# A linear attention's division moved off its matmul result: query features as the moving operand, reciprocals spread over the partitions by DMA

## The chip, the core and the metric

The kernel runs on one core of a Trainium2 chip. The metric is the device time of one execution in microseconds, the median of several runs. The core has five engines with instruction queues of their own: PE (TensorE, matmuls), DVE (VectorE), ACT (ScalarE), POOL (GpSimd) and SP (SyncE, which here only issues DMAs). Each executes its queue strictly in order; between engines the program waits on semaphores.

## The reference

Three stages follow each other. All data are float32; heads have S = 576 tokens of 64 numbers, there are 4 batches of 8 heads.

```
proj = x @ w_phi                         # x = q or k of a head: 576 x 64 -> 576 x 128
proj = proj - max(abs(proj), axis=-1)
phi  = concat(exp(proj), exp(-proj))     # 576 x 256 features
kv   = phi(k).T @ v                      # 256 x 64
z    = sum over tokens of phi(k)         # 256
num  = phi(q) @ kv                       # 576 x 64
den  = phi(q) @ z + 1e-6                 # 576
attention = num / den                    # all heads side by side: x, 2304 tokens x 512

h = x @ w_in; g = h * clip(h + 3, 0, 6) / 6; x = g @ w_out      # 512 -> 2048 -> 512
expert = argmax(x @ w_gate)              # one of 8 for each token
out = gate * sigmoid(x @ w_output_gate)[expert] * (relu(x @ w1[expert]) @ w2[expert])
```

## The kernel before, in words

**Attention.** Two heads are a pair; there are 16. The queries and keys of a pair come as one array with the head dimension on partitions. A pair's tokens are 9 tiles of 128: 8 main tiles and one tail tile that holds the last 64 tokens of both heads. They are treated in groups (GROUPS): group 0 is the tail tile, groups 1 and 2 have 4 tiles each. For each group PE projects q and k (line 726), DVE takes the absolute maximum, its negative (the bias) and the difference for the query side (lines 1256, 1258, 1262), ACT takes the key's exponentials (L1073, `k_features`), PE transposes the query's differences (L740), and ACT takes their exponentials (L1059, `q_features`), so that query features have features on partitions. PE multiplies v and key features (L753, `kv_sums`) to a 64 x 256 result per head, ACT copies it (L1083), PE transposes it (L761). POOL adds up the tiles of key features (L555, L571, `sums_first` and `sums_second`), and PE sums them over partitions by a product with ones (L769, `z_sums`). ACT copies kv and z (L1089, `copy_kv`).

The numerators (L781, and L790 for the tails) have a tile of query features as the stationary operand and kv with z beside it as the moving one: the result has tokens on partitions, and column 64 of a tile is its denominator. DVE (`normalise`, L1269 to L1281) adds 1e-6, takes the reciprocal and multiplies from PSUM into x_sb, again with tokens on partitions. PE's numerators of the next pair wait for that (`x_ready`).

The pairs are software-pipelined. `both(u)` on every engine holds the later part of pair u and the projections of pair u + 1 (DVE: u + 1 and u + 2). In POOL's `both(u)` the order is: last additions of pair u, in pairs 8 to 15 a piece of the MLP's weights, first additions of pair u + 1. In PE's: transposes, `kv_sums`, projections of group 0 of the next pair, transposes, `z_sums`, projections of group 1, half of the numerators and tails, projections of group 2, the rest of the numerators. ACT's `k_features` of group 0 of pair u + 1 waits for the sums of pair u (`pk_summed`), because it overwrites their input.

SP's loop for pair u (`next_pair`) loads the queries and keys of pair u + 2 (L362), its v (L368, L370), waits until DVE has searched (`piece_max`) or split (`piece_lo`) the current pieces of the MLP's weights, and loads the next two pieces of 512 KB (`load_pieces`, L375, L378). After pair 7 it issues 8 stores of padding rows (L414). All of these are DMAs of one queue. Pair 7 has extra steps on DVE for the maximum of the MLP's weights.

**MLP.** Weights and x are split into two half-precision parts, a high and a low one, and three products are summed. 2304 tokens are 18 tiles, in 6 blocks of 3. Block n needs x with features on partitions (`xt`). ACT and DVE write the parts with tokens on partitions (`x_hi`, `x_lo`; L1100, L1418); block 0's are transposed by PE in the last pair (L703, 24 transposes, copied by L1108), the others by DMA (`turn_x`, 3 DMAs a block). The tail tokens need three DMAs that move them to other partitions. During the MLP the expert weights are loaded (`load_unit`, L427), searched on DVE (L1483), split and stored.

**Experts.** The MLP's rows are scattered to a buffer ordered by expert and worked off in slots of 128 rows. The first three slots belong to the expert with most tokens among the first four blocks.

## Time and profile before

| | us |
|---|---|
| median of 3 runs | 861.37 (860.11 to 865.08) |
| profiled execution | 863.49 |
| its span, first to last instruction | 861.7 |
| attention, to the first MLP matmul | 208.84 |
| PE busy | 827.6 |
| DVE busy | 572.5 |
| ACT busy | 383.6 |
| POOL busy | 180.2 |

The granted clock of PE is 0.995 of full speed over the span. A row of the timeline is: start, duration, engine (SPq is SP's queue, PEld a weight load), line, operation, tiles, count, and in brackets the idle time of the engine before it with what ended it. Float32 matmuls have two records each.

### The profile page before, as it was taken

The page shows a single profiled execution, that of the slowest core. Times are in us where ns is not written, and L with a number is a line of the kernel's source. Part 1 is how long each engine was busy: PE and PEld are TensorE (multiplying, and loading weights), DVE is VectorE, ACT ScalarE, POOL GpSimd, SP SyncE. Part 2 cuts the span into 40 slices and gives each one's busy share as a digit, 9 for nine tenths or more (in the row PEclk, how much of TensorE's full clock was granted, in tenths as well). Part 3 has the DMA queues.
Part 4 walks back from the last instruction along what each step waited for, and adds up shares of the span by engine and source line. Part 5 has one row for each costly group of instructions (what it writes and reads, how often), then busy time and mean ns, then how long its engine had stood idle before and what let it go on. Part 6 is the DMA issues. An engine that isn't in the chain of part 4 may idle for free.

```text
span 861.7 us, 19310 instructions
## 1 busy us (share of the span) xinstructions
PE 827.6 (96%) x7018; PEld 549.2 (64%) x7019; DVE 572.5 (66%) x1200; ACT 383.6 (45%) x798; POOL 180.2 (21%) x208
## 2 busy tenths in 40 slices
PE   7999999999999999999999999999899999999995
PEld 5888777876555555555455555556577767777773
DVE  4778788877887998998898898855532444222221
ACT  5766667776555555555555555523111111111110
POOL 4444376663000001001001001010121222111100
PEclk9999999999999999999999999999999999999998
DMA  7255565541483884875784875485253852656610
GB/s 223 98 178 180 166 205 181 177 136 61 172 286 132 267 257 173 267 258 172 256 256 183 256 256 183 162 300 193 92 182 139 313 197 76 238 201 219 233 70 14
DMA packets 76554, 163.83 MB, mean 190 GB/s; under 512 B 39574, under 2 KB 43926, under 8 KB 69840
## 3 DMA queue, kind: packets, MB, share of 16 engines
q1 hardware_dynamic: 70576, 146.20, 50.3%
q0 software_dynamic: 5760, 16.80, 5.7%
q8 instruction: 35, 0.57, 0.3%
q14 instruction: 23, 0.19, 0.1%
q10 hardware_dynamic: 160, 0.07, 0.0%
HBM read 109.44 MB, written 47.47 MB: 182 GB/s over the span
## 4 chain that ended last, share of the span: by engine, by line
PE 70%; DVE 12%; issue 6%; DMA 5%; ACT 3%; POOL 2%; another core or an unknown queue 1%; DVEq 0%; POOLq 0%; ACTq 0%; SPq 0%
PE ps L876 18%; PE ps L865 15%; PE ps L971 11%; PE ps L959 11%; DMA arena<-split 4%; PE ps L781 4%; PE ps L726 3%; PE ps L753 3%; ACT arena L1073 2%; DVE arena L1256 2%; DVE arena L1510 2%; POOL arena L555 1%; PE ps L740 1%; DVE yrow L1475 1%; DVE relu L1566 1%
## 5 line engine op out<-in xcount | busy, mean ns | idle before, releaser
L865 PE MATMUL ps<-arena,w_in_sb 128*128 128x384 f16 x1152 | 200.9, 326 | 0.0
L876 PE MATMUL ps<-w_out_sb,arena 128*128 128x512 f16 x576 | 171.2, 379 | 5.0 <-DVE stage L1571 4.9
L865 PEld LDWEIGHTS ps<-arena,w_in_sb 128*128 128x128 f16 x1152 | 112.3, 98 | 80.9
L959 PE MATMUL ps<-x_sb,arena 128*128 128x128 f16 x2112 | 121.7, 219 | 3.9 <-DMA arena<-split 3.0
L959 PEld LDWEIGHTS ps<-x_sb,arena 128*128 128x128 f16 x2112 | 119.3, 98 | 8.1 <-issue 4.9
L1233 ACT ACTIVATE x_sb<-ps 128x512 f16<-128x512 f32 x54 | 31.6, 596 | 206.7 <-PE ps L959 172.4
L971 PE MATMUL ps<-arena,x_sb 128*128 128x512 f16 x528 | 119.7, 383 | 2.2 <-DVE x_sb L1667 2.2
L876 PE MATMUL ps<-w_out_sb,stage 128*128 128x512 f16 x288 | 109.1, 379 | 0.0
L1073 ACT ACTIVATE arena<-ps,arena 128x128 f32<-128x128 f32 x288 | 79.4, 382 | 55.4 <-DVE arena L1258 51.2
L1205 ACT ACTIVATE arena<-relu 128x384 f16<-128x384 f32 x96 | 50.0, 521 | 109.5 <-DVE relu L1566 108.3
L876 PEld LDWEIGHTS ps<-w_out_sb,arena 128*128 128x128 f16 x576 | 55.8, 98 | 65.4 <-issue 7.2
L1667 DVE SCALAR_TENSOR_TENSOR x_sb<-ps,x_sb 128x512 f16<-128x512 f32 x54 | 36.7, 689 | 85.1 <-ACT x_sb L1233 83.1
L1194 ACT ACTIVATE relu<-ps,three,s_h 128x384 f32<-128x384 f32 x96 | 63.6, 663 | 60.9 <-PE ps L865 60.4
L971 PEld LDWEIGHTS ps<-arena,x_sb 128*128 128x128 f16 x528 | 51.0, 99 | 60.3 <-ACT x_sb L1233 2.6
L1510 DVE SCALAR_TENSOR_TENSOR arena<-arena,u_up 128x1024 f16<-128x1024 f32 x64 | 79.3, 1280 | 6.3 <-ACT arena L1182 5.6
L555 POOL TENSOR_TENSOR arena<-arena 128x512 f32<-128x512 f32 (+1 forms) x64 | 63.9, 998 | 79.9 <-ACT arena L1073 73.2
L1483 DVE TENSOR_REDUCE u_mx<-arena 128x1 f32<-128x1024 f32 x64 | 74.8, 1208 | 1.5 <-DMA arena<-in_moe_w 1.5
L1182 ACT ACTIVATE arena<-arena,u_up 128x1024 f16<-128x1024 f32 x64 | 72.5, 1140 | 3.4 <-DVE u_up L1502 2.2
L610 POOL PARTITION_ALL_REDUCE u_all<-u_red x16 | 7.8, 489 | 314.7 <-DVE u_red L1487 314.7
L1566 DVE SCALAR_TENSOR_TENSOR relu<-relu,ps 128x384 f32<-128x384 f32 x96 | 52.7, 549 | 26.8 <-ACT relu L1194 25.2
L1256 DVE TENSOR_REDUCE arena<-ps 128x8 f32<-128x1024 f32 (+1 forms) x48 | 45.8, 955 | 35.3 <-PE ps L726 34.4
L1677 DVE TENSOR_SCALAR x_sb<-ps,stage 128x512 f32<-128x512 f32 x27 | 20.2, 748 | 69.9 <-PE ps L971 69.9
(210 smaller groups left out, 976.9 us busy)
## 6 DMA issues: line engine op xcount, KB each, us to landing
arena<-split SPq DMA_DIRECT2D x36, 1024.0 KB
arena<-in_moe_w SPq DMA_DIRECT2D x16, 2048.0 KB
split<-arena SPq DMA_DIRECT2D x16, 2048.0 KB, 7.5
arena<-in_qkt SPq DMA_DIRECT2D x15, 576.0 KB, 6.2
stage<-in_moe_w_in SPq DMA_DIRECT2D x16, 512.0 KB, 4.1
stage<-in_moe_w_out SPq DMA_DIRECT2D x16, 512.0 KB, 5.3
x_sb<-rows POOLq DMA_DIRECT2D x27, 257.0 KB
arena<-in_v SPq DMA_DIRECT2D x32, 128.0 KB, 4.4
```

Source lines behind the costliest of these rows:

```text
L555: nc.gpsimd.tensor_tensor(out, x, y, ALU.add).then_inc(sum_step, 1)
L865: last = nc.tensor.matmul(ps[:, HB[f % GB], 0:BN], w_in_sb[:, lw, c, f * P:(f + 1) * P], xt[:, a, lx, c, :], start=c == 0 and lw + lx == 0 ...
L876: last = nc.tensor.matmul(ps[:, YB + r, :], g_sb[lg_][:, f % GB, r * P:(r + 1) * P], w_out_sb[:, lw, f, :], start=f == 0 and lg_ + lw == 0 ...
L959: last = nc.tensor.matmul(ps[:, bank, f % 4 * P:(f % 4 + 1) * P], w1_sb[b][:, lw, c, f * P:(f + 1) * P], xgt[:, a, lx, c, :], start=c == 0 ...
L971: last = nc.tensor.matmul(ps[:, 6 + a, :], hg[:, a, lh, f, :], w2_sb[b][:, lw, f, :], start=f == 0 and lh + lw == 0, stop=f == EFC - 1 and ...
L1073: last = nc.scalar.activation(pk[:, t0 + t, s, :], ps[:, bank, t * F:(t + 1) * F], ACT.Exp, bias=bias[:, t0 + t:t0 + t + 1], scale=1.0 - 2 ...
L1182: nc.scalar.activation(split_sb[:, 0, q_ * Q:(q_ + 1) * Q], raw[b][:, q_ * Q:(q_ + 1) * Q], ACT.Copy, scale=u_up[:, b:b + 1]).then_inc(u_h ...
L1194: nc.scalar.activation(relu3[:, f % GB, :], ps[:, HB[f % GB], 0:BN], ACT.Relu, bias=three[:, 0:1], scale=s_h[:, 0:1]).then_inc(relu3_ready, 1)
L1256: nc.vector.tensor_reduce(mx[:, j:j + 2, t0:t0 + n], src, AX.X, ALU.max, apply_absolute_value=True).then_inc(max_ready, 1)
L1483: nc.vector.tensor_reduce(u_mx[:, q_:q_ + 1], raw[b][:, q_ * Q:(q_ + 1) * Q], AX.X, ALU.max, apply_absolute_value=True).then_inc(u_searche ...
L1510: nc.vector.scalar_tensor_tensor(out=split_sb[:, 1, cols], in0=raw[b][:, cols], scalar=u_up[:, b:b + 1], in1=split_sb[:, 0, cols], op0=ALU ...
L1566: nc.vector.scalar_tensor_tensor(out=relu3[:, f % GB, :], in0=relu3[:, f % GB, :], scalar=6.0, in1=ps[:, HB[f % GB], 0:BN], op0=ALU.min, o ...
```

## The change: what it does

Seven things, in the words of the diff:

1. Queries are laid out so that the query features of a head are contiguous in token order, and `numerators` has kv (64 columns of a head) as the stationary operand and 320 or 256 tokens as the moving one. The result has a head's 64 features on partitions; the two heads of a pair fill 128 partitions.
2. `denominators` computes the 1152 denominators of a pair with z, repeated in 32 columns, as the stationary operand: four groups of 32 partitions, two banks of 144 tokens.
3. ACT (`copy_low`) and DVE (`copy_high`) copy numerators and denominators undivided from PSUM to SBUF, x into `x_t`, where features are on partitions.
4. SP moves the denominators to 128 partitions x 9 (`den_over`); DVE takes the reciprocals (`reciprocals`, one pair later); SP stores them to DRAM (`rec_out`) and loads them back, repeated over 64 partitions for each head (`rec_in`). Their order in SP's loop is in the diff.
5. POOL multiplies x of pair u - 2 by them in place (`normalise`) between the two additions in `both(u)`; DVE does the last two pairs in block 0 of the MLP.
6. The MLP's parts of x are written straight from `x_t` to `xt`; PE's transposes, `turn_x`, the moves of the tails and their waits go.
7. Tokens are in natural order in the tiles; SP loads the first two units of expert weights after the last numerators.

```diff
--- before.py
+++ after.py
...
+LOW, HIGH = TAIL + 2 * P, 2 * P
+QUARTER = S // 4
+REP, ZW = 32, 2 * DH + 64
 GROUPS = [(8, 1), (0, 4), (4, 4)]
 TILES = N // P
-MAIN = B * MT
...
-        x_sb = sb("x_sb", [P, MAIN + B, DM])
+        x_t = sb("x_t", [P, DC, N])
+        x_flat = x_t[:].rearrange("p c n -> p (c n)")
+        den_sb = sb("den_sb", [P, 2, 2 * QUARTER])
+        rec = sb("rec", [P, 2, PT])
...
+        rec_wide = yrow_words[:].rearrange("p r d -> p (r d)")[:, 0:2 * S].rearrange("p (a n) -> p a n", a=2)
...
+        def x_of(u, k, n):
+            return x_flat[:, bass.ds(u % DC * N + u // DC * S + k, n)]
...
+            def held(x):
+                return x if isinstance(x, int) else sp.snap(x)
+
+            def rec_out(i, k, a):
+                u, made = held(i * 2 + k), held(i * 2 + (k + 1))
+                sp.wait_ge(rec_made, made)
+                sp.dma_start(recs[bass.ds(u, 1), :].rearrange("o (p t) -> (o p) t", t=PT), rec[:, a, :]).then_inc(rec_stored, 16)
+
+            def den_over(i, a):
+                copied = held(i * 2 + (a + 1))
+                sp.wait_ge(low_copied, copied)
+                sp.wait_ge(high_copied, copied)
+                sp.dma_start(rec[:, a, :], den_sb[0:P:REP, a, :].rearrange("g (i t) -> g i t", t=PT)).then_inc(den_moved, 16)
+
+            def rec_in(i, k, a):
+                u, stored_by = held(i * 2 + k), held(i * 32 + (k * 16 + 16))
+                sp.wait_ge(rec_stored, stored_by)
+                if isinstance(u, int) and u == PAIRS - 1:
+                    sp.wait_ge(x_ready, PAIRS - 2)
+                for hh in range(2):
+                    sp.dma_start(rec_wide[DH * hh:DH * hh + DH, a, :],
+                                 recs[bass.ds(u, 1), S * hh:S * hh + S].to_broadcast([DH, S])).then_inc(rec_loaded[a], 16)
...
+            def first_phase(i, a):
+                later = not isinstance(i, int) or i * 2 + a > 0
+                next_pair(i, a)
+                if later:
+                    rec_out(i, a - 1, 1 - a)
+                den_over(i, a)
+                sp.wait_ge(piece_max, i * 2 + (a + 1))
+                if isinstance(i, int) and i == PAIRS // 4 - 1:
+                    load_pieces(0, a, a)
+                else:
+                    load_pieces(i + 1, a, i * 2 + (a + 2))
+                if later:
+                    rec_in(i, a - 1, 1 - a)
...
+                    rec_out(i, a - 1, 1 - a)
+                    den_over(i, a)
                     sp.wait_ge(piece_lo, i * 2 + (a + 1 - PAIRS // 2))
                     load_pieces(i - (PAIRS // 4 - 1), a, i * 2 + (a + 2 - PAIRS // 2))
+                    rec_in(i, a - 1, 1 - a)
+            for a in range(2):
+                rec_out(PAIRS // 2 - 1, a - 1, 1 - a)
+                den_over(PAIRS // 2 - 1, a)
+                rec_in(PAIRS // 2 - 1, a - 1, 1 - a)
...
-            sp.wait_ge(x_ready, PAIRS)
-            load_unit(0, 0, 0)
-
-            sp.dma_start(x_sb[TAIL:P, MAIN, :], x_sb[0:TAIL, MAIN + 1, :]).then_inc(tails_moved, 16)
-            sp.dma_start(x_sb[TAIL:P, MAIN + 1, :], x_sb[0:TAIL, MAIN + 3, :]).then_inc(tails_moved, 16)
-            sp.wait_ge(tails_moved, 32)
-            sp.dma_start(x_sb[0:TAIL, MAIN + 1, :], x_sb[0:TAIL, MAIN + 2, :]).then_inc(tails_moved, 16)
-            load_unit(0, 1, 1)
-            def turn_x(n):
-
-                sp.wait_ge(xs_hi, n + 1)
-                sp.wait_ge(xs_lo, n + 1)
-                if n > 1:
-                    sp.wait_ge(h_done, (n - 1) * FC)
-                for r in range(BT):
-                    sp.dma_start_transpose(xt[:, n % 2].rearrange("p l c n -> p (l c) n")[:, :, r * P:(r + 1) * P],
-                                           xs[:, r].rearrange("p l d -> p (l d)")).then_inc(xt_turned, 16)
+            sp.wait_ge(num_done, PAIRS)
+            for m in range(2):
+                load_unit(0, m, m)
+            rec_out(PAIRS // 2 - 1, 1, 1)
+            rec_in(PAIRS // 2 - 1, 1, 1)
...
+            def normalise(u, a):
+                pool.wait_ge(rec_loaded[a], (u - a) * 16 + 32)
+                nc.gpsimd.tensor_tensor(x_of(u, 0, S), x_of(u, 0, S), rec_wide[:, a, :], ALU.mult).then_inc(x_ready, 1)
...
                 sums_second(u)
                 if phase:
                     piece_hi_of(u, a)
+                if not isinstance(u, int) or u > 1:
+                    normalise(u - 2, a)
                 sums_first(u + 1)
...
-                        c = (2 * s + 1) * P + DH * hh
-                        last = nc.tensor.matmul(ps[:, KVB, c:c + DH], pk_sum[:, hh, s, :], ones[:, 0:DH], start=True, stop=True)
+                        c = s * ZW + P + REP * hh
+                        last = nc.tensor.matmul(ps[:, KVB, c:c + REP], pk_sum[:, hh, s, :], ones[:, 0:REP], start=True, stop=True)
...
+            def numerators(bank, k, n):
                 for s in range(2):
                     for hh in range(2):
-                        c = 2 * MT * P + DH * hh
-                        nc.tensor.matmul(ps[DH * hh:DH * hh + TAIL, NB, TAIL_AT:TAIL_AT + 2 * DH], pq[:, s, c:c + TAIL], kv_of(s, hh),
+                        c = S * hh + k
+                        nc.tensor.matmul(ps[DH * hh:DH * hh + DH, bank, 0:n], kv_sb[:, s, DH * hh:DH * hh + DH], pq[:, s, c:c + n],
                                          start=s == 0, stop=s == 1)
+
+            def denominators():
+
+                for b in range(2):
+                    for s in range(2):
+                        for g in range(4):
+                            c = 2 * g * QUARTER + b * QUARTER
+                            z = P + REP * (g // 2)
+                            last = nc.tensor.matmul(ps[REP * g:REP * g + REP, NB + b, DEN_AT:DEN_AT + QUARTER], kv_sb[:, s, z:z + REP],
+                                                    pq[:, s, c:c + QUARTER], start=s == 0, stop=s == 1)
+                return last
...
                 pe.wait_ge(pq_ready, u * 3 + 2)
                 if not isinstance(u, int) or u > 0:
-                    pe.wait_ge(x_ready, u)
-                numerators(u, range(2))
-                numerator_tails(u)
+                    pe.wait_ge(low_copied, u)
+                    pe.wait_ge(high_copied, u)
+                numerators(NB, 0, LOW)
                 if more:
                     projections(u + 1, 1 - a, 2)
-                else:
-                    for c in range(DC):
-                        x_transpose(c, X0[c])
                 if top is not None:
                     max_turn(*top)
                 pe.wait_ge(pq_ready, u * 3 + 3)
-                last = numerators(u, range(2, MT))
+                numerators(NB + 1, LOW, HIGH)
+                last = denominators()
...
+            def copy_low(u, a):
+                act.wait_ge(num_done, u + 1)
+                if not isinstance(u, int) or u > 0:
+                    act.wait_ge(den_moved, u * 16)
+                nc.scalar.copy(x_of(u, 0, LOW), ps[:, NB, 0:LOW])
+                nc.scalar.copy(den_sb[:, a, 0:QUARTER], ps[:, NB, DEN_AT:DEN_AT + QUARTER]).then_inc(low_copied, 1)
...
                 k_features(u + 1, 1 - a, 0)
+                if not isinstance(u, int) or u > 0:
+                    copy_low(u - 1, 1 - a)
                 copy_kv(u)
...
                 copy_kvt(u)
-                x_hi(0)
+                copy_low(u - 1, 0)
                 copy_kv(u)
                 q_features(u, 2)
-                for c in range(DC):
-                    copy_xt(c, X0[c])
+                x_hi(0, 0)
                 piece_hi_of(u, 1)
+                copy_low(u, 1)
...
+            def copy_high(u, a):
                 dve.wait_ge(num_done, u + 1)
-                num = ps[:, NB:NB + 2, 0:MT * NW].rearrange("p h (t d) -> p h t d", t=MT)
-                nc.vector.tensor_scalar(den[:, a, 0:2 * MT].rearrange("p (h t) -> p h t", h=2), num[:, :, :, DH], 1e-6, None, ALU.add)
-                nc.vector.tensor_scalar(den[:, a, 2 * MT:PT], ps[:, NB, TAIL_AT + DH:TAIL_AT + NW], 1e-6, None, ALU.add).then_inc(den_step, 1)
-                dve.wait_ge(den_step, u * 2 + 1)
-                nc.vector.reciprocal(den[:, a], den[:, a]).then_inc(den_step, 1)
-                dve.wait_ge(den_step, u * 2 + 2)
-                for hh in range(2):
-                    rows_ = slice(DH * hh, DH * hh + TAIL)
-                    last = nc.vector.tensor_tensor(x_sb[0:TAIL, bass.ds(b + MAIN, 1), bass.ds(j * P + hh * DH, DH)].rearrange("p o d -> p (o d)"),
-                                                   ps[rows_, NB, TAIL_AT:TAIL_AT + DH],
-                                                   den[rows_, a, 2 * MT:PT].to_broadcast([TAIL, DH]), ALU.mult)
-                last.then_inc(tails_ready, 1)
-                for hh in range(2):
-                    last = nc.vector.tensor_tensor(x_sb[:, bass.ds(b * MT, MT), bass.ds(j * P + hh * DH, DH)], num[:, hh, :, 0:DH],
-                                                   den[:, a, MT * hh:MT * hh + MT, None].to_broadcast([P, MT, DH]), ALU.mult)
-                last.then_inc(x_ready, 1)
+                nc.vector.tensor_copy(den_sb[:, a, QUARTER:2 * QUARTER], ps[:, NB + 1, DEN_AT:DEN_AT + QUARTER])
+                nc.vector.tensor_copy(x_of(u, LOW, HIGH), ps[:, NB + 1, 0:HIGH]).then_inc(high_copied, 1)
+
+            def reciprocals(u, a):
+                dve.wait_ge(den_moved, u * 16 + 16)
+                nc.vector.tensor_scalar(rec[:, a, :], rec[:, a, :], 1e-6, None, ALU.add).then_inc(den_step, 1)
+                dve.wait_ge(den_step, u + 1)
+                nc.vector.reciprocal(rec[:, a, :], rec[:, a, :]).then_inc(rec_made, 1)
 
             def pair_out(u, a):
-                normalise(u, a, u // (H // 2), u % (H // 2))
+                copy_high(u, a)
+                if not isinstance(u, int) or u > 0:
+                    reciprocals(u - 1, 1 - a)
+
+            def normalise(u, a):
+                dve.wait_ge(rec_loaded[a], (u - a) * 16 + 32)
+                dve.wait_ge(low_copied, u + 1)
+                nc.vector.tensor_tensor(x_of(u, 0, S), x_of(u, 0, S), rec_wide[:, a, :], ALU.mult).then_inc(x_last, 1)
...
+                        reciprocals(PAIRS - 1, 1)
+                    if f == 3 and not post:
+                        normalise(PAIRS - 2, 0)
+                    if f == 4 and not post:
+                        normalise(PAIRS - 1, 1)
...
```

## Rows read from the trace of the kernel before

**Rows 1.** Engine table of the page: busy time, share of the span, instructions.

```profile
PE 827.6 (96%) x7018; PEld 549.2 (64%) x7019; DVE 572.5 (66%) x1200; ACT 383.6 (45%) x798; POOL 180.2 (21%) x208
```

**Rows 2.** Windows: length, busy time (count) of PE, PEld, DVE, ACT, POOL, clock, DMA.

```profile
48.00:60.00 12.00, 12.00 (x120) 9.97 (x118) 9.56 (x21) 8.34 (x29) 5.49 (x6) 1.00 0.50 166
```

**Rows 3.** Timeline of one pair: start, duration, engine, line, idle time before.

```profile
86.73 1.27 POOL L571 TENSOR_TENSOR arena<-arena 128x512 f32<-128x512 f32 x1 [0.17 <-POOL arena L555]
89.09 1.16 PE L726 MATMUL ps<-wphi_sb,arena 64*128 64x128 f32 x16
91.79 2.17 ACT L1073 ACTIVATE arena<-ps,arena 128x128 f32<-128x128 f32 x8 [1.02 <-DVE arena L1258]
94.03 2.88 POOL L555 TENSOR_TENSOR arena<-arena 128x512 f32<-128x512 f32 x3 [6.04 <-ACT arena L1073]
98.50 1.27 POOL L571 TENSOR_TENSOR arena<-arena 128x512 f32<-128x512 f32 x1 [0.16 <-POOL arena L555]
99.91 0.62 ACT L1073 ACTIVATE arena<-ps,arena 128x128 f32<-128x128 f32 x2 [0.72 <-DVE arena L1258]
```

**Rows 4.** Timeline of POOL: three of the 16 last additions, pairs 2, 8, 15.

```profile
38.96 1.27 POOL L571 TENSOR_TENSOR arena<-arena 128x512 f32<-128x512 f32 x1 [0.17 <-POOL arena L555]
113.48 1.28 POOL L571 TENSOR_TENSOR arena<-arena 128x512 f32<-128x512 f32 x1
199.54 1.27 POOL L571 TENSOR_TENSOR arena<-arena 128x512 f32<-128x512 f32 x1
```

**Rows 5.** Groups of PE by form, 0 to 235 us: busy, mean ns, idle.

```profile
L781 PE MATMUL ps<-arena 128*128 128x128 f32 x512 | 65.6, 281 | 0.7 <-issue 0.7
L753 PE MATMUL ps<-arena 128*64 128x256 f32 x320 | 40.7, 394 | 2.1 <-ACT arena L1073 1.8
```

**Rows 6.** Groups of ACT by form, 0 to 235 us: copies out of PSUM.

```profile
L1083 ACT COPY arena<-ps 128x256 f32<-128x256 f32 x16 | 6.1, 383 | 0.7 <-PE ps L753 0.7
L1089 ACT COPY arena<-ps 128x512 f32<-128x512 f32 x16 | 9.4, 585 | 5.7 <-PE ps L769 5.7
```

**Rows 7.** Timeline of SP: the two weight loads of one pair.

```profile
89.31 0.33 SPq L375 DMA_DIRECT2D stage<-in_moe_w_in  x1
89.84 0.38 SPq L378 DMA_DIRECT2D stage<-in_moe_w_out  x1
```

**Rows 8.** DMA issues from 84 to 100 us: KB each, median us to landing.

```profile
arena<-in_qkt SPq DMA_DIRECT2D x1, 576.0 KB, 7.2
stage<-in_moe_w_in SPq DMA_DIRECT2D x1, 512.0 KB, 4.0
stage<-in_moe_w_out SPq DMA_DIRECT2D x1, 512.0 KB, 4.8
```

**Rows 9.** Group of DVE by form, 0 to 235 us: the division's first product.

```profile
L1276 DVE TENSOR_TENSOR x_sb<-ps,arena 64x64 f32 x20 | 4.4, 221 | 4.4 <-DVE arena L1272 4.3
```

**Rows 10.** Landing times of the three moves of tail tokens, minimum first.

```profile
DMA to landing us min/median/max: 2.2/8.3/8.5
```

**Rows 11.** Timeline around the padding stores: SP, then PE's next group 0.

```profile
106.67 5.33 SPq L414 DMA_DIRECT2D rows<-relu  x8
112.39 0.35 SPq L362 DMA_DIRECT2D arena<-in_qkt  x1
125.83 0.49 PE L726 MATMUL ps<-wphi_sb,arena 64*128 64x128 f32 x4
```

**Rows 12.** DMA issues from 104 to 128 us, the features of pair 10.

```profile
arena<-in_qkt SPq DMA_DIRECT2D x1, 576.0 KB, 10.8
```

**Rows 13.** Timeline from the last pair to the MLP's block 0.

```profile
200.54 1.59 ACT L1100 ACTIVATE yrow<-x_sb,s_up 128x1536 f16<-128x1536 f32 x1
202.16 1.82 DVE L1418 SCALAR_TENSOR_TENSOR yrow<-x_sb,s_up,yrow 128x1536 f16<-128x1536 f32 x1
208.84 6.01 PE L865 MATMUL ps<-arena,w_in_sb 128*128 128x384 f16 x36
219.72 2.35 DVE L1483 TENSOR_REDUCE u_mx<-arena 128x1 f32<-128x1024 f32 x2 [1.50 <-DMA arena<-in_moe_w]
```

More of the change, by code:

```diff
@@ L71, with moe_program @@
 NOWHERE = 2 * N
-def moe_program(nc, qkt_in, v, w_phi, w_in, w_out, w_gate, w_ogate, w1, w2, out, rows, split):
+def moe_program(nc, qkt_in, v, w_phi, w_in, w_out, w_gate, w_ogate, w1, w2, out, rows, split, recs):
     ctx = ExitStack()
@@ L913, in mlp_block @@
                 first = isinstance(n, int) and n == 0
[L914 to L917 removed]
+                pe.wait_ge(xs_hi, n + 1)
+                pe.wait_ge(xs_lo, n + 1)
+                if first:
+                    pe.wait_ge(consts_made, 2)
                     pe.wait_ge(piece_hi, PAIRS // 2 - 1)
@@ L930, in mlp_block @@
                         hidden(n, a, f + 2)
-                    if first and f == 0:
-                        pe.wait_ge(x_ready, PAIRS)
                     if not more and f == FC - 1:
@@ L1796 @@
     split = nc.dram_tensor("split", (E, 2, P, 2 * UW), F16, kind="Internal").ap()
-    moe_program(nc, *args, out, rows, split)
+    recs = nc.dram_tensor("recs", (PAIRS, 2 * S), F32, kind="Internal").ap()
+    moe_program(nc, *args, out, rows, split, recs)
     r = _run(nc, [arrays], core_ids=[0])
```

128 lines of the change are left out of this document (46 added, 82 removed).

## The prediction

> **What bounds the kernel now.** The page's engine table comes first: TensorE is busy 96% of the span [rows 1]. In a window of steady attention (48 to 60 us) it is busy all 12.00 us, and POOL (GpSimd) only 5.49 [rows 2]. That reads as "TensorE bounds, POOL is free". The timeline of one pair corrects it [rows 3]. Follow a loop through four engines: projections of group 1 start on PE at 89.09, VectorE reduces them and makes the bias, ScalarE takes exponentials at 91.79 (2.17 us), POOL adds from 94.03 almost without a pause until 98.50 + 1.27 = 99.77, PE's ones-matmuls wait for these sums, and the next projections are queued behind them. From one such POOL row to the next is 98.50 - 86.73 = 11.77 us, the period of a pair. So two loops are equally long: PE's own work, and this one, whose tail, 94.03 to 99.77 = 5.74 us of POOL additions, nothing shortens. POOL's idle time (6.04 us before 94.03) is not spare room of the loop; it is only spare for work whose input is there.
>
> I call S(p) the end of pair p's last POOL addition (line 571): S(2) = 40.23, S(8) = 114.76, S(15) = 200.81 [rows 4]. The 13 periods between first and last take 160.6 us: 12.4 each, the slow seventh (weights' maximum) included.
>
> **The change part by part.**
>
> *PE, numerators.* Removed are 32 + 8 matmul records a pair. The 512 of line 781 took 65.6 us busy [rows 5], 4.1 a pair, and the tails 0.6. Added: 16 records with 64 output partitions, 320 and 256 columns. Line 753 has that shape with 256 columns: 320 records in 40.7 us [rows 5], 0.127 each with its waits, about 0.104 without (20 in 2.07 us), because the two column halves run beside each other. So 8 x 0.104 x 320/256 = 1.04 and 8 x 0.104 = 0.83 us. The denominators are 32 records of 144 columns with 32 output partitions, a form the trace doesn't have: between 0.93 us (four beside each other) and 3.8 us (0.118 each, as line 781). I take 1.3, near the half-width form. PE thus gives back 4.7 - 3.2 = 1.5 us a pair. It is worth nothing here: the loop of rows 3 doesn't contain the numerators, and the projections of group 2, queued behind them, wait for VectorE's difference of group 1 anyway (3.3 us after the start of group 1).
>
> *VectorE* drops the division (about 2 us a pair) for two copies and two tiny operations (about 1.1 us). *ScalarE* gains two copies from PSUM, 320 and 144 columns: by 0.383 for 256 and 0.585 for 512 columns [rows 6] about 0.43 + 0.29, overlapped 0.55 us.
>
> *POOL* gains a product of 576 columns over all partitions: 1.27 x 576/512 = 1.43 us. By length it fits the idle 6.04 us. But POOL executes in order, and the product waits for its reciprocals. Behind it are queued the additions of the next pair, so the loop now runs through these steps, from S(p), with the pair p-2 as passenger:
> 1. ScalarE's exponentials of group 0 of pair p+1 wait for pair p's sums: at 99.91 for S = 99.77, 0.62 long [rows 3]. Behind them, in order, copy_low of p-1: done at S + 1.25 (0.14 + 0.56 + 0.55).
> 2. SP waits for that copy before it moves the denominators of p-1 (den_over). Wake 0.15, one issue 0.6: S + 2.0.
> 3. Only then, in SP's order, come the two loads of MLP weights, 0.53 us apart as at 89.31 and 89.84 [rows 7]: S + 2.05 and S + 2.6. (Their own wait, for VectorE's search, ended at S + 1.15, no longer decides.)
> 4. Only then the two broadcasts of the reciprocals of p-2 (rec_in), issued at S + 3.2 and S + 3.8.
> 5. They go to the queue of the weights. Landings in one period: first weights 4.0, second 4.8, query/key features, issued 0.6 later still, 7.2 us after their issues [rows 8], that is at 93.3, 94.6 and 97.6: order of issue, 512 KB in 1.3 us. So the broadcasts (295 KB) land about 0.9 us behind the second weights: 2.6 + 4.8 + 0.95 = S + 8.35.
> 6. Product 1.43 and 0.1 of gaps, then 5.74 of additions: S(p+1) = S(p) + 15.6.
>
> The Trainium skill ("DMA: Bandwidth & Descriptors", section "Queues, rings and completion order") says that each DMA engine consumes the descriptors of a ring in their order and that SP has one ring on each engine; the trace's landings agree. [...]
>
> While the addresses are computed from a loop counter an instruction waits longer: 0.43 us before line 1276 after its wait (4.3 us over 10 looped pairs [rows 9]). That holds for POOL's product in pairs 2 to 7: 16.0 there. Bounds of the landing: below, a broadcast that overtakes the weights and takes the shortest landing seen after its issue, 2.2 us [rows 10]: S + 6.0, period 13.2; above, 2 us more for two transfers at half rate to half the partitions: 17.6. I take order of issue, since three landings show it.
>
> 6 x 16.0 + 7 x 15.6 = 205.2 against 160.6: +44.6. The seventh pair's search delay (3.2 us) falls into the new slack.
>
> *The padding stores.* After pair 7 SP issues 8 stores (5.33 us) and then, from 112.39, the load of pair 10's features, which lands after 10.8 us at 123.2; PE used it at 125.83 [rows 11, 12]. Weights of that step were issued at 105.7, so the load lands 17.5 us after them. Now these weights are issued at S(8) + 2.05 and the broadcasts come too: landing at S(8) + 20.3, where PE wants it at S(8) + 10.5, and the copy that SP waits for comes at S(8) + 22.6 instead of S(9) + 1.25 = S(8) + 16.9. Once, +6 us (0 if the queue drains faster, 8 at most).
>
> *The end of attention.* Before: S(15) = 200.81 to the first MLP matmul at 208.84 [rows 13], 8.0 us. The 24 transposes go. Now ScalarE does the last exponentials until S + 2.75 (1.1 of ones-matmuls, 0.5 copy, 1.1), the half-precision part of x 1.59 (row at 200.54), VectorE the rest 1.82 (row at 202.16): matmuls from S + 6.3, -1.7. But SP loads the first expert weights after rec_in of pair 14, whose reciprocals VectorE makes behind its part of x: S + 11.0 instead of 10.0. VectorE wants them relative to the MLP's start, in block 0; they came at 219.72 after a wait of 1.5 [rows 13]. So 2.7 later in relation, and about 2.4 of it passes to PE: +2.4. Sum +0.7 (-1.7 to +4).
>
> *MLP and experts.* Parts of x are written in place by the same two operations; 15 transposing DMAs go, but no PE wait of the MLP is put down to them: 0 (down to -3). Token order changes; by the reference's own argmax the same expert comes first with 384 early tokens and 22 slots run in either order: 0.
>
> **Sum.** 44.6 + 6 + 0.7 = +51.3 on the profiled execution's 863.5 us (span 861.7): 914.8. The median of the runs lies 2.1 below that execution: 913.
>
> **Rivals.**
> A, broadcasts aren't held by the weights: period 13.2 (13.6 looped), so 6 x 13.6 + 7 x 13.2 = 174 against 160.6, +13.4, +6, +0.7: 881. For it: many packets of several transfers are in flight; the small broadcasts use few. Against it: the three landings.
> B, not slower: the wait on the reciprocals stays inside POOL's idle time. That decides at S + 4.5 (94.03 - 88.00 - 1.5). Then the loop stays 11.8 to 12.1, the late VectorE start in pairs 8 to 14 (about 0.3 each) goes and the end gains: 863.5 - 2 - 1.7, median 858. For it: 6 us of idle POOL. Against: the broadcasts are issued only at S + 3.2 to 3.8 and the shortest landing is 2.2.
> C, the narrow denominators don't overlap, 3.8 us, and the reciprocals are early: PE's loop is 11.5 - 4.5 + 1.9 + 3.8 + 1.2 (the wait for group 1) = 13.9, 13 times 1.6 more: 882. Beside the main case this is hidden.
>
> **How the numbers follow.** Forecast 0.64, A 0.18, B 0.10, C 0.04, slower still than the range 0.04. The forecast's own range: landing 1.5 us to either side over 13 pairs, without the padding part below: 888 to 934. Taking A in: 874 to 934. Within 0.5% of no change (4 us) is what a measurement can't tell apart; B lies at its edge, half faster, half same: 0.06 and 0.05; slower 0.89.
>
> **What would show it.** In the changed profile: POOL's additions at line 571 about 15.6 us apart; POOL idle before the product, released by a DMA from recs into yrow; those broadcasts landing 4.5 to 5 us after issue, behind the weights; PE idle some 4 us a pair before the ones-matmuls; a longer period at pair 9. The narrow denominators' time a record shows the PE term. It is wrong if the product starts right after the additions of its pair, or if the periods are under 13.

## The result, and the profile after

The changed kernel is slower: 943.26 us median of 4 runs (938.04 to 951.37) against 860.83 (860.11 to 865.08) of the kernel before beside it, ratio 1.0959 [1.0914, 1.1004]. The forecast was 913, the range 874 to 934: the direction was right, the size was not, and the range did not hold it. The profiled execution took 951.37 us, its span is 949.7.

The engine table of the page, which answers to [rows 1]:

```profile
PE 850.7 (90%) x7122; PEld 541.5 (57%) x7123; DVE 561.6 (59%) x1154; ACT 388.2 (41%) x826; POOL 205.2 (22%) x219
```

The timeline of POOL, last additions of pairs 2 and 15, which answers to [rows 4]:

```profile
38.54 1.28 POOL L602 TENSOR_TENSOR arena<-arena 128x512 f32<-128x512 f32 x1 [0.17 <-POOL arena L586]
274.94 1.26 POOL L602 TENSOR_TENSOR arena<-arena 128x512 f32<-128x512 f32 x1
```

S(2) is 39.82 and S(15) 276.20: 236.4 us where it was 160.6. So 75.8 of the 88.0 us by which the span grew lie between these two rows. The first MLP matmul comes 7.9 us after S(15) (8.0 before). The MLP takes 393.6 us to the first expert matmul (387.0), the experts 272.0 (265.9); the last 6 us belong to this execution, the slowest of the four, since e4 below, with the same expert stage, takes 266.1.

The timeline of one pair, from S(6) = 111.35 on, which answers to [rows 3] and [rows 7]:

```profile
111.47 0.62 ACT L1095 ACTIVATE arena<-ps,arena 128x128 f32<-128x128 f32 x2 [5.45 <-POOL arena L602]
112.29 0.30 ACT L1118 COPY den_sb<-ps 128x144 f32<-128x144 f32 x1
112.61 0.62 SPq L410 DMA_DIRECT2D rec<-den_sb  x1
113.44 0.35 SPq L381 DMA_DIRECT2D stage<-in_moe_w_in  x1
113.98 0.39 SPq L384 DMA_DIRECT2D stage<-in_moe_w_out  x1
114.56 1.84 SPq L418 DMA_DIRECT2D yrow<-recs  x2
119.59 1.19 PE L811 MATMUL ps<-arena 128*32 128x144 f32 x32
121.09 1.43 POOL L613 TENSOR_TENSOR x_t<-x_t,yrow 128x576 f32 x1 [9.74 <-DMA yrow<-recs]
122.46 2.89 POOL L586 TENSOR_TENSOR arena<-arena 128x512 f32<-128x512 f32 x3
126.93 1.26 POOL L602 TENSOR_TENSOR arena<-arena 128x512 f32<-128x512 f32 x1 [0.16 <-POOL arena L586]
```

POOL ends its additions, sits 9.74 us until a DMA, multiplies, and then adds for the next pair without a pause. PE, which was busy without a gap in [rows 2], waits 4.6 us for POOL's sums in this pair, and ACT 5.5; over 12 pairs these waits are 51.3 and 59.5 us. For POOL's product the whole stage is one line, what it waited for (us, times):

```profile
  DMA yrow<-recs: 118.7, 13
```

The DMA issues of that pair (113 to 122 us: KB each, median us to landing), which answer to [rows 8]:

```profile
arena<-in_qkt SPq DMA_DIRECT2D x1, 576.0 KB, 5.4
stage<-in_moe_w_in SPq DMA_DIRECT2D x1, 512.0 KB, 4.1
stage<-in_moe_w_out SPq DMA_DIRECT2D x1, 512.0 KB, 5.8
yrow<-recs SPq DMA_DIRECT2D x2, 144.0 KB, 4.9
```

### The profile page after: what moved, and what is told of

The parts are those of the page before. It is cut to its first block, busy times and chain, and to the rows that moved or that the text cites. A ratio compares the mean times of both kernels' runs of the same rounds, so it can differ in the third digit from the quotient of the medians.

```text
span 949.7 us, 19633 instructions
## 1 busy us (share of the span) xinstructions
PE 850.7 (90%) x7122; PEld 541.5 (57%) x7123; DVE 561.6 (59%) x1154; ACT 388.2 (41%) x826; POOL 205.2 (22%) x219
## 4 chain that ended last, share of the span: by engine, by line
PE 51%; issue 13%; DVE 12%; POOL 12%; DMA 6%; ACT 2%; SPq 2%; another core or an unknown queue 1%; POOLq 0%; ACTq 0%; DVEq 0%
PE ps L896 13%; PE ps L979 11%; PE ps L991 11%; PE ps L885 11%; POOL arena L586 7%; DMA yrow<-recs 3%; DVE arena L1533 3%; DVE u_mx L1506 2%; POOL w_in_sb L608 2%; POOL arena L602 2%; DVE relu L1589 2%; DMA arena<-split 2%; PE ps L969 1%; POOL x_t L613 1%; DMA arena<-in_moe_w 1%
## 5 line engine op out<-in xcount | busy, mean ns | idle before, releaser
L979 PE MATMUL ps<-x_t,arena 128*128 128x128 f16 x2112 | 125.0, 222 | 6.8 <-DMA arena<-split 3.6
L979 PEld LDWEIGHTS ps<-x_t,arena 128*128 128x128 f16 x2112 | 122.7, 100 | 11.5 <-issue 8.6
L991 PE MATMUL ps<-arena,x_t 128*128 128x512 f16 x528 | 119.6, 382 | 2.1 <-DVE x_t L1695 2.1
L1258 ACT ACTIVATE x_t<-ps 128x512 f16<-128x512 f32 x54 | 31.6, 596 | 212.8 <-PE ps L979 182.4
L1695 DVE SCALAR_TENSOR_TENSOR x_t<-ps,x_t 128x512 f16<-128x512 f32 x54 | 36.7, 689 | 91.2 <-ACT x_t L1258 90.1
L991 PEld LDWEIGHTS ps<-arena,x_t 128*128 128x128 f16 x528 | 50.8, 98 | 59.8 <-ACT x_t L1258 2.5
L750 PE MATMUL ps<-wphi_sb,arena 64*128 64x128 f32 x576 | 59.0, 355 | 16.9 <-DMA arena<-in_qkt 8.0
L586 POOL TENSOR_TENSOR arena<-arena 128x512 f32<-128x512 f32 (+1 forms) x64 | 70.0, 1093 | 13.9 <-ACT arena L1095 6.4
L793 PE MATMUL ps<-ones,arena 128*128 128x32 f32 x128 | 25.8, 359 | 51.3 <-POOL arena L602 51.3
```

The source lines that it names most:

```text
L586: nc.gpsimd.tensor_tensor(out, x, y, ALU.add).then_inc(sum_step, 1)
L750: done = nc.tensor.matmul(ps[:, bank, t * F:(t + 1) * F], qkt[DH * w:DH * w + DH, a, c:c + P], wphi_sb[DH * w:DH * w + DH, :], start=True, ...
L979: last = nc.tensor.matmul(ps[:, bank, f % 4 * P:(f % 4 + 1) * P], w1_sb[b][:, lw, c, f * P:(f + 1) * P], xgt[:, a, lx, c, :], start=c == 0 ...
L991: last = nc.tensor.matmul(ps[:, 6 + a, :], hg[:, a, lh, f, :], w2_sb[b][:, lw, f, :], start=f == 0 and lh + lw == 0, stop=f == EFC - 1 and ...
```

## The experiments

The kernel before ran beside each of them, at 857.2 to 860.0 us median. "Period" is the distance from one S to the next.

**Which order of the queue?** e1 issues the broadcasts right behind the store of the reciprocals, ahead of den_over and the weights; e3 behind den_over, ahead of the weights.

```diff
                 if later:
                     rec_out(i, a - 1, 1 - a)
+                    rec_in(i, a - 1, 1 - a)      # e1
                 den_over(i, a)
+                rec_in(i, a - 1, 1 - a)          # e3
                 ... (weights)
-                    rec_in(i, a - 1, 1 - a)
```

> Only SP's order is changed: the two broadcasts of a pair's reciprocals are issued right after their store, before the denominators of the next pair and before the MLP's weights, about 6 us ahead of the end of POOL's additions. Queue theory (POOL waits in order for broadcasts that SP issues too late and that queue behind 1 MB of weights): POOL's wait for the broadcasts goes from 118.7 us in all to under 5, its additions at line 602 are again 11.8 to 12.3 us apart, once about 6 more behind the padding stores; attention ends near 216 to 222 instead of 284, total 870 to 880. Clock theory (the long periods come from PE at half clock): the order of DMAs hardly matters, total over 930. Work theory (the product itself, 1.42 us on POOL, and the two copies on ScalarE lengthen the loop): periods of 13.5 and more, total over 895.

> Only SP's order is changed, less far than in the first: the broadcasts are issued after the denominators and before the two weight loads (S + 2.1 instead of S + 3.2, with S the end of the last addition), so nothing large is in the queue ahead. If being queued behind the weights is the larger part of the lateness they land 3.3 to 3.8 us after the first issue, near S + 5.7, and the period is 13 to 14 us, total 880 to 895. If the broadcasts are slow by themselves (64 reads of one DRAM row, half of the partitions each) they still take 5 to 6 us to land, S + 7.5, and the period is near 15, total 905.

Measured: e1 887.6 us, ratio 1.033 [1.031, 1.036]; e3 894.3, 1.041 [1.039, 1.043]. In both, SyncE's order alone brings back 49 to 56 us. e3 is as expected: the period is 13.4 to 13.7 us in the first half. The rows of e3 for the pair with S = 94.39:

```profile
96.48 1.18 SPq L418 DMA_DIRECT2D yrow<-recs  x2
97.84 1.04 SPq L381 DMA_DIRECT2D stage<-in_moe_w_in  x1
100.70 1.42 POOL L613 TENSOR_TENSOR x_t<-x_t,yrow 128x576 f32 x1 [6.32 <-DMA yrow<-recs]
```

The product starts at S + 6.3 and not at S + 9.7. Over the 12 regular pairs (2 to 14 without 9) the second broadcast is issued 1.4 us earlier than in the changed kernel (S + 2.9 for 4.2) and lands 3.2 us after its issue instead of 5.9: these 2.7 us are what the weights in front cost. The period is near that of rival A (13.6 in looped pairs), by another order. e1 missed its expectation, and so did both theories' figures: the period is 12.2 to 14.6 us outside the slow seventh and pair 9. The waits for the broadcasts fall from 118.7 to 40.2 us and not under 5, because SyncE can't send them 6 us ahead of S: VectorE has made the reciprocals only 1 to 3 us before S, their store takes 1.8 us to land, and the broadcasts go out at S - 1.2 to S + 0.8. So in the first half the product still starts at S + 2.9 to 5.6, and there it meets VectorE's work for group 1. The timeline of the pair with S = 78.19:

```profile
83.02 1.40 POOL L612 TENSOR_TENSOR x_t<-x_t,yrow 128x576 f32 x1 [4.82 <-DMA yrow<-recs]
83.14 1.29 DVE L1282 TENSOR_SCALAR arena<-arena 128x4 f32<-128x4 f32 x1
84.47 2.18 ACT L1094 ACTIVATE arena<-ps,arena 128x128 f32<-128x128 f32 x8 [2.16 <-DVE arena L1282]
85.08 1.98 PE L749 MATMUL ps<-wphi_sb,arena 64*128 64x128 f32 x16 [2.05 <-DVE arena L1286]
```

VectorE's bias of four columns takes 0.17 us elsewhere and 1.29 beside GpSimd's product; it ends when the product ends, and it stands in the loop that feeds GpSimd's additions: they start 2.3 us after the product's end in 8 of the 13 pairs. The Trainium skill ("SBUF — State Buffer", section "Who interferes with whom") says that VectorE and GpSimd share a pair of ports as an exclusive lock and that, beside a VectorE operation in a mode with two ports, the engine that issues later "fully blocks". These two rows agree with the lock; the mode of the operation isn't in the profile.

**Is it the additions queued behind the wait?** e2 leaves SyncE's order and puts POOL's product behind the first additions of the next pair. e7 leaves SyncE's order too and gives the product to VectorE, behind its reciprocals.

```diff
-                    normalise(u - 2, a)
                 sums_first(u + 1)
+                    normalise(u - 2, a)      # e2 (e7: in VectorE's pair_out)
```

> Only POOL's order is changed: the product of pair u - 2 stands behind the first three additions of pair u + 1 instead of ahead of them. The broadcasts come as late as before (9.7 to 11.1 us after the end of the last addition). Queue theory: the 2.9 us of additions now run inside the wait, so the period falls by about that, from 18.2 to 15.0 to 15.5, total 900 to 910. Clock theory: no change, 935 to 950.

> The changed kernel (943 us) with only the product moved from GpSimd to VectorE; SyncE's order is left, so the broadcasts still land 9.7 to 11.1 us after the end of the additions. Theory 1 (the loss comes from the additions queued on GpSimd behind a product that waits): the additions no longer wait, but VectorE now waits for the broadcasts in order, at the end of its pair, about 12 us after the additions; the period becomes 12 to 13 and the time 865 to 885. Rival 2 (the loss is the late transfer, whoever multiplies): VectorE's bias and difference of group 0 of the next pair are queued behind the product, and the period stays at 16 or more, 920 or more.

Measured: e2 901.7 us, 1.047 [1.044, 1.051], periods 13.4 to 15.2, at pair 9 21.9; e7 883.4, 1.029 [1.027, 1.032], S(2) to S(15) 177.4 us. Both times lie where the theory of the queued additions had them. In e7 not one DMA is issued earlier in its pair: the broadcasts still go out 3.2 us after S, behind the weights, but only VectorE waits for them, late in its pair, 5.1 us in all:

```profile
93.12 1.97 SPq L418 DMA_DIRECT2D yrow<-recs  x2
95.92 2.88 POOL L586 TENSOR_TENSOR arena<-arena 128x512 f32<-128x512 f32 x3 [6.02 <-ACT arena L1088]
99.48 1.37 DVE L1305 TENSOR_TENSOR x_t<-x_t,yrow 128x576 f32<-128x576 f32 x1 [0.40 <-DMA yrow<-recs]
```

So about 60 of the 82 us hang on the product's wait and its time standing ahead of the additions, on an engine that works in order; e2, which leaves the product on GpSimd and only puts the next pair's first additions ahead of it, gets back 42 of them. POOL's idle time before the additions is 6.02 us again, as in [rows 3].

**Is it TensorE's clock?** The granted clock of the changed kernel is 0.94 over the span. Windows of two pairs show it; 0.78 is the mean of stretches at the full level, 2.4 GHz, and at the half one (length, busy time and count of PE, PEld, DVE, ACT, POOL, clock, DMA share, GB/s):

```profile
93.09:111.35 18.26, 13.68 (x123) 9.49 (x123) 8.79 (x16) 8.61 (x28) 6.61 (x7) 0.78 0.40 123
111.35:128.19 16.84, 13.16 (x123) 9.40 (x123) 10.89 (x17) 8.61 (x28) 6.63 (x7) 0.85 0.45 134
```

e4 adds 14 products of the identity, read by nobody, in each pair while TensorE waits for the sums.

```diff
+                for _ in range(14):
+                    nc.tensor.matmul(ps[:, KVB, 2 * ZW:512], ident[:], ident[:], start=True, stop=True)
                 pe.wait_ge(pk_summed, u + 1)
```

> Everything as in the changed kernel, but PE runs 14 matmuls that nobody reads (float32, 128 columns) before it waits for POOL's sums in each pair, so that it rests about 1 us instead of 4 to 5. The granted clock should stay at 1.0 in attention. Clock theory: periods fall from 18.2 to 14 or less, total under 900. Queue theory: the loop through POOL holds no PE work except before the last addition of pairs 8 to 14, so the periods fall by at most 1 us, total 925 to 943, part of it the half-clock stretch at the MLP's start (3.4 us).

Measured: 942.1 us, 1.096 [1.094, 1.098], as the changed kernel. The window of the same pair:

```profile
98.11:115.49 17.38, 14.18 (x153) 10.77 (x152) 8.79 (x16) 8.56 (x28) 6.61 (x7) 1.00 0.45 130
```

The clock is at its full 2.4 GHz level over that pair and the period is 17.4 us. The product still starts at S + 9.0 to 11.8. From pair 3 on, e4's periods sum to 213.7 us against 218.4: without the falls to 1.2 GHz this stretch is 4.7 us shorter, net of what the added records cost there; they cost 4.1 us in pairs 0 to 2, where TensorE doesn't wait (S(3) is 61.9 for 57.8). The falls are a result of the waits, not their cause.

**Was TensorE's time worth nothing before?** e8 is the kernel before with half of the numerators' records left out.

```diff
-                        for s in range(2):
-                            last = nc.tensor.matmul(..., pq[:, s, c:c + P], kv_of(s, hh), start=s == 0, stop=s == 1)
+                        last = nc.tensor.matmul(..., pq[:, 0, c:c + P], kv_of(0, hh), start=True, stop=True)
```

> The kernel before, with half of the numerator matmuls left out (only the first of the two halves of the features is summed, for queries outside the tail), so the output isn't the reference's and only the attention stretch is compared. 16 records a pair less are 2.0 us of TensorE's time. If the loop through GpSimd's additions bounds the kernel before (the prediction's claim that time given back by TensorE is worth nothing), the periods between the ends of the additions stay at 11.7 to 12.0 us outside the slow seventh. If TensorE's own work bounds it (96% busy), they fall to about 10 us.

Measured: the periods are 11.8, 12.1, 11.8, 12.1, 11.8 us where they were 11.8, 12.1, 11.8, 12.1, 11.8, and S(2) to S(15) is 160.4 us for 160.6. TensorE is 96% busy in the kernel before, and 2 us a pair less of its work give nothing here. (The whole takes 863.7 us, 857.3 beside it; with another output it isn't compared.) That leaves the loop of [rows 3], through VectorE, ScalarE and the additions, as the bound of the stage.

**Both repairs, and the rest.** e5 has e1's order and e7's product. e6 also issues the padding stores four and four behind the loads of pairs 10 and 11, and the last pair's broadcasts between the two expert loads.

```diff
-            for e in range(E):
-                sp.dma_start(rows[e * REGION:e * REGION + P, :], zrow).then_inc(pads_stored, 16)
+            for a in range(2):
+                second_phase(PAIRS // 4, a)      # loads, reciprocals and weights of one pair
+                pads(range(4 * a, 4 * a + 4))
...
             load_unit(0, 0, 0)
-            load_unit(0, 1, 1)
             rec_out(PAIRS // 2 - 1, 1, 1)
             rec_in(PAIRS // 2 - 1, 1, 1)
+            load_unit(0, 1, 1)
```

> The changed kernel with the broadcasts issued directly behind the store of the reciprocals (as in e1, 887.6 us) and with the product taken from GpSimd and given to VectorE, behind its reciprocals of the pair. Theory 1 (GpSimd's product costs twice: it waits in order ahead of the additions, and while it runs VectorE's small operations crawl, 1.29 us instead of 0.17): both go, the period of a pair falls from e1's 13.8 us to that of the kernel before, 11.8 to 12.2, plus the padding stores; 13 periods take 153 to 165 us and the kernel 862 to 872. Rival 2 (the period of e1 is set by TensorE and ScalarE, whose work grew, and GpSimd's product is hidden): the period stays at 13 or more, since VectorE now has 0.75 us a pair more, and the time is 885 or more.

> As e5, with the eight padding stores issued four and four behind the two pairs after the half instead of ahead of them, and the last pair's reciprocals stored and spread behind the first expert load instead of both. If the padding stores delay the load of the features of pair 10 and cost about 6 us once, the period after the ninth pair is no longer some 6 us longer than its neighbours, and the time is 5 to 7 us under e5. If the stores only move the delay to another pair, the two are equal within 2 us.

Measured: e5 878.0 us, 1.024 [1.020, 1.027]; e6 872.0, 1.019 [1.014, 1.024]. e5 lies 6 us above the range of its theory, with 174.3 us from S(2) to S(15) for 153 to 165. Its regular period is 12.2 to 12.5 us and the one after pair 9 is 22.9 (TensorE waits 8.6 us for the features behind the padding stores; in e6 4.2 us, one pair later). e6 saved the 6 us it was to save, but not as its theory had it: the long period moved to pair 10 and is 18.9 us; one of its four runs took 879.0. The timeline of e5 has the rest:

```profile
95.25 2.88 POOL L585 TENSOR_TENSOR arena<-arena 128x512 f32<-128x512 f32 x3 [6.01 <-ACT arena L1087]
98.29 1.88 POOL L585 TENSOR_TENSOR arena<-arena 128x512 f32<-128x512 f32 x1 [0.16 <-POOL arena L585]
98.33 0.71 DVE L1304 TENSOR_TENSOR x_t<-x_t,yrow 128x576 f32<-128x576 f32 x1
```

The same collision the other way round: the addition that meets VectorE's product takes 1.88 us instead of 1.27, and it is in the loop. By these rows it started 0.04 us before the product, so they don't show that the later one waits. e9 therefore multiplies right after VectorE's difference of group 1, where GpSimd is idle, takes the first search (or piece) of the weights behind the copies, spreads the padding stores one a pair behind the broadcasts, and puts an expert load ahead of the last reciprocals' store.

```diff
                 differences(u + 1, 1 - a, 1)
-                piece(u, a, 0)
+                product(u - 2, a)
                 differences(u + 1, 1 - a, 2)
                 pair_out(u, a)
+                piece(u, a, 0)
                 differences(u + 2, a, 0)
```

> All steps at other places, the computation that of the changed kernel: VectorE multiplies right after the difference of group 1 (where GpSimd has nothing to do) and takes its first search of the weights behind the pair's copies; the eight padding stores go one a pair, behind the broadcasts; the first expert load ahead of the last denominators. In e5 and e6 the period was 12.4 us where the kernel before has 11.8 to 12.1, because one of GpSimd's additions took 1.88 us instead of 1.27 while VectorE's product ran. Theory 1 (the two engines hinder each other only while both run such operations): periods of 11.8 to 12.1 us, no long period after the ninth or tenth pair, S(2) to S(15) about 161 to 163 us, the first MLP matmul at 205 to 210 us, and 855 to 862 us, level with the kernel before or up to 3 us under it. Rival 2 (12.4 is set by the transfers or by ScalarE's two more copies): periods stay at 12.3 to 12.5, 866 or more.

Measured: 877.2 us, 1.022 [1.021, 1.024], a miss as a whole, with two parts. In the first half the periods from pair 2 are 11.7, 12.1, 13.4, 12.1, 11.7 (ahead of the 13.4 TensorE waits 1.1 us for the features). In the second they are 12.6 to 14.5, and the MLP starts badly; its rows:

```profile
127.88 2.02 DVE L1333 SCALAR_TENSOR_TENSOR w_in_sb<-stage,s_up,w_in_sb 128x1024 f32 x1
128.90 2.13 POOL L607 TENSOR_TENSOR arena<-arena 128x512 f32<-128x512 f32 x1
227.77 0.67 ACT L1217 ACTIVATE relu<-ps,three,s_h 128x384 f32<-128x384 f32 x1 [12.67 <-DMA rows<-relu]
```

The moved piece of the weights now meets the last addition (2.02 and 2.13 us for 1.27 each), and the last padding store came late. e10 takes these places back; e12 moves the padding stores behind the pair's loads of values.

```diff
                     next_pair(i, a)
+                    pad(i, a)                    # e12
                     rec_out(i, a - 1, 1 - a)
                     rec_in(i, a - 1, 1 - a)
-                    pad(i, a)                    # e9, e10
                     den_over(i, a)
```

> As e9 (877 us), with three of its places taken back. In e9 the periods of the first half were 11.7 to 12.1 us, but 12.6 to 13.0 in the second half, where VectorE's 1024-column piece of the weights had moved beside GpSimd's additions (2.02 and 2.13 us instead of about 1.2 and 1.27), and the MLP's first activation waited 12.7 us for the last padding store. So in the second half the piece is back ahead of the difference of group 2 and VectorE multiplies behind the pair's copies, two padding stores go ahead of the second half and six one a pair, and the expert load goes behind the last broadcasts, as in e6. Theory 1 (a collision of VectorE and GpSimd, and the place of the padding stores, are all that is left over the kernel before): periods of 11.8 to 12.1 in the first half and 12.1 to 12.3 in the second, S(2) to S(15) about 162 to 164 us, the time 857 to 863, within 0.7% of the kernel before. Rival 2 (the queue's load, not places, makes the long periods): at least one period of the second half stays 4 us over its neighbours, and the time is 867 or more.

> As e10 (870 us, ratio 1.015), with each padding store issued behind the pair's loads of values, in the stretch in which the DMA engines are idle, and not behind the broadcasts, ahead of the weights and the features; the first two in pairs 6 and 7. In e10 TensorE waited 1.2 to 1.9 us for the features (in_qkt) in each pair of the second half, and the periods there were 12.5 to 15.2. Theory (the order of the bytes ahead of the features, not their number, makes these waits): the waits for in_qkt go, the periods of the second half are 12.1 to 12.4, S(2) to S(15) 161 to 164 us, the time 860 to 865. Rival (the padding bytes cost this wherever they stand in the second half): the periods stay at 13 and the time at 868 or more.

Measured: e10 870.5 us, 1.015 [1.013, 1.018]; e12 866.7, 1.0095 [1.007, 1.012]. In e12 S(3) to S(7) is 51.97, 64.10, 75.86, 87.93, 99.71 and in the kernel before 52.00, 64.14, 75.92, 88.00, 99.77: with the product in GpSimd's idle time the first half is back to the kernel before. In the second half, where VectorE's piece of the weights has that place back, the periods are 12.2 to 13.2 against 12.1. There the product still meets an addition (1.66 us), and the wait for the features is smaller but not gone:

```profile
137.45 1.44 DVE L1309 TENSOR_TENSOR x_t<-x_t,yrow 128x576 f32 x1 [0.25 <-issue]
138.35 1.66 POOL L608 TENSOR_TENSOR arena<-arena 128x512 f32<-128x512 f32 x1
139.69 0.49 PE L749 MATMUL ps<-wphi_sb,arena 64*128 64x128 f32 x4 [1.01 <-DMA arena<-in_qkt]
```

In e10 the first half was as well 11.8 to 12.1 us, the second 12.5 to 15.2 with a wait for the features in each pair: each theory was right for one half. S(2) to S(15) is 168.7 us in e10 and 164.6 in e12, for 160.6 in the kernel before: the order of these bytes took half of the excess back, and e12 ends just above its expectation (1.7 us over it in the time). Of the 5.5 us by which its span exceeds the kernel before's, only 2.0 lie ahead of the first MLP matmul; 3.6 lie in the MLP. No version beats the kernel before: e12 is 0.95% over it.

## Why the prediction was wrong in size

The mechanism was the one forecast: GpSimd's product waits in order for broadcasts that stand behind the weights, and the additions wait behind the product. What failed is the size of one term, the landing in step 5, and a part of step 6. By its own steps, read at the 12 regular pairs (2 to 14 without 9), landings read issue by issue:

Steps 1 to 4 came as written. den_over is issued at S + 1.26 and is over at 1.9 (forecast 2.0), the weights go at S + 2.1 and 2.65 (2.05 and 2.6), the first broadcast at S + 2.9 to 3.7 (3.2). The second broadcast goes at S + 3.4 to 5.7, mean 4.2 (3.8).

**Step 5 failed: the landing of the second weights.** The broadcasts have landed at S + 9.0 to 11.1, mean 10.10, and not at S + 8.35. The step took 4.8 us from the issue of the second weights to their landing, and 0.95 for the broadcasts behind them. Measured are 6.35 us (5.5 to 7.2), so the weights land at S + 8.95 instead of 7.4, and 1.15 us more for the broadcasts. So 1.55 of the missing 1.75 us a pair are the first term. Its 4.8 us were one landing, the shortest of the kernel before, whose median was 5.3, in a queue without broadcasts. The range gave the landing 1.5 us to either side, up to S + 9.85, and the mean lies beyond that. The upper bound of the step (2 us more, period 17.6) comes near the number, but nothing shows the half rate that it was made of.

That standing behind the weights costs this time is shown by e3. The order of issue, on which the step rested, holds only in part: in the pair shown the first broadcast lands at 119.62, ahead of the second weights (119.75), and the first load of values, issued behind the features, at 121.86, ahead of them (122.02). The kernel before had such a case already, in the same pair as [rows 8]: the values at 96.2, the features issued ahead of them at 97.6. How much of the 1.55 us comes from the broadcasts behind the weights, and why the second weights take 5.5 to 5.8 us in some pairs and 6.2 to 7.2 in the others, stays open: a kernel that holds the features back until the broadcasts have landed wasn't tried.

The 0.43 us of register time came as forecast: in the looped pairs 2 to 7 the product starts 0.41 to 0.48 us after the landing, in pairs 8 to 14 0.07 us after it.

**Step 6** held in the first half: from the start of the product to the next S 6.9 to 7.5 us (forecast 7.27). In the second half, from pair 10 on, it is 7.8 (8.7 at the end), because a 1024-column piece of the weights on VectorE now falls into GpSimd's additions, which have no idle time between them but take longer. Four of them take 4.23 us in pair 8, without such a piece beside them, and 5.07 in pair 11:

```profile
157.37 4.23 POOL L586 TENSOR_TENSOR arena<-arena 128x512 f32<-128x512 f32 x4
216.06 5.07 POOL L586 TENSOR_TENSOR arena<-arena 128x512 f32<-128x512 f32 x4
217.50 1.72 DVE L1330 SCALAR_TENSOR_TENSOR w_out_sb<-stage,s_up,w_out_sb 128x1024 f32 x1
```

The balance of S(2) to S(15): forecast +44.6 and +6 for the padding stores, 50.6; measured 75.8, so 25.2 are missing. Landing 12 x 1.75 = 21.0, from landing to product +0.4, step 6 -0.8 in pairs 2 to 8 and +3.5 from pair 10 on, the period at pair 9 22.15 against 21.6, +0.5: 24.6. The rest is rounding in the forecast.

**The padding term** came near (22.15 us, 4.6 over the mean of its neighbours, 16.6 and 18.4; forecast 6), by the mechanism given: TensorE waited for the features of pair 10.

```profile
165.28 0.80 PE L750 MATMUL ps<-wphi_sb,arena 64*128 64x128 f32 x4 [5.81 <-DMA arena<-in_qkt]
```

**The end and the MLP.** S(15) to the first MLP matmul was to be 6.3 us and is 7.9, at a granted clock of 0.57 (mostly 1.2 GHz); in e5, without these waits, it is 6.0. The late expert load was priced at 2.4 us, and the MLP is 6.6 longer in this trace and 4.5 in e1; the row that answers to the last of [rows 13] has a wait of 4.92 us instead of 1.50:

```profile
298.65 2.34 DVE L1506 TENSOR_REDUCE u_mx<-arena 128x1 f32<-128x1024 f32 x2 [4.92 <-DMA arena<-in_moe_w]
```

**PE's term** was near: 1.78 us (1.30 in e5, at full clock) and 1.08 for the numerators, 1.19 for the denominators; forecast 1.04, 0.83 and 1.3. Rival C falls with it. Rival B falls with the 118.7 us of waits. Rival A falls too: the first broadcast overtook the second weights in 9 of the 12 pairs, but the product needs both, and the second broadcast never did. Not being held by the weights is what e3 makes by hand.

Of 87.9 us between the two profiled executions the forecast had 51.3. The other 36.6, up to rounding: 25.2 in the loop, 1.6 at its end, 4.2 in the MLP, 6.1 in the experts of this one execution, -0.4 ahead of pair 2.

The prediction missed one mechanism altogether: what GpSimd's and VectorE's operations do to each other. In the first half of the changed kernel it costs little, because the product ran while VectorE was mostly idle (the bias is 0.17 us, at most 0.50); in the second half it is the +3.5 us above, and it decided once the wait was gone, in e1, e5 and e9. Its sign stood in the trace of the kernel before: the same piece of VectorE took 1.27 us alone and 1.77 to 1.85 beside GpSimd's L577.

## What to carry to other kernels

An engine with idle time is free only for work whose input is there: put ahead of work that a loop waits for, one late operand stops the loop, and moving that single instruction (e7, -60 us) was worth no less than moving its data (e1, -56, and e3, -49 us). A landing time read from one pair of a quieter queue is a lower bound where transfers are added; take the loaded rows, or the upper end. And where GpSimd adds in a critical loop, place VectorE's products of two inputs and its small operations in GpSimd's gaps, not beside its work.

## What the hardware showed that was not expected

- A 128 x 4 TENSOR_SCALAR of VectorE took 0.17 us alone and 1.29 (up to 1.41) beside a 1.40 us TENSOR_TENSOR of GpSimd; an addition of GpSimd took 1.27 us alone, 1.66 to 1.88 beside a 576-column product of VectorE and 2.13 beside its 1024-column piece, which itself took 2.02 us for 1.27. VectorE's TENSOR_REDUCE of 1024 columns kept its 1.21 to 1.23 us beside GpSimd's additions.
- 32 denominator matmuls with 32 output partitions and 144 columns took 1.19 us at full clock, 0.037 each, where a record of [rows 5] with 128 output partitions and 128 columns takes 0.128: as if four ran beside each other.
- A broadcast of 144 KB landed 2.8 to 3.2 us after its issue in most pairs of e1, ahead of the pair's loads of 512 KB, and 4.4 to 7.1 us after it in the changed kernel, behind them. One issued behind a load of 512 KB landed before it (119.62 and 119.75), so landings don't keep the order of issue on one queue.
